# Softmax finished in its selection's step, and filling matmuls, in a fused attention, MLP and expert kernel

## The reference, cut to what matters

```python
def _attn_ref(q, k, v):                        # batch 4, 8 heads, 576 rows, head 64
    scores = scale * np.matmul(q, k.transpose(0, 1, 3, 2))
    kth = np.partition(scores, -32, axis=-1)[..., -32:-31]
    scores = np.where(scores >= kth, scores, -1000000000.0)
    attn = np.exp(scores - np.max(scores, axis=-1, keepdims=True))
    attn = attn / (np.sum(attn, axis=-1, keepdims=True) + 1e-09)
    return np.matmul(attn, v)

def _moe_ref(x, w_in, w_out):                  # 2304 tokens, 512 -> 2048 -> 512
    h = x @ w_in
    return (np.maximum(h, 0.0) + np.log1p(np.exp(-np.abs(h)))) @ w_out

def _moe2_ref(x, w_gate, w1, w2):              # best of 8 experts for each token, 512 -> 1024 -> 512
    ...
    ye = np.maximum(xe @ w1[e], 0.0) @ w2[e]
    out[mask] = gate_w[mask, None] * ye
```

## Time and profile before

| | |
|---|---|
| median of 3 runs | 1057.04 us (1056.1 to 1057.84) |
| the profiled execution | 1057.04 us |
| its span | 1054.8 us |
| mean granted clock of TensorE | 0.983 |
| busy: TensorE, VectorE, ScalarE, GpSimd | 992.9, 817.3, 727.6, 711.9 us |
| HBM | 123 GB/s over the span |

### The profile page before, as it was taken

How to read it: one execution, slowest core, us unless ns; L and a number is a source line. 1 busy time by engine, 2 the same in 40 slices (tenths; PEclk the granted TensorE clock), 3 DMA queues, 4 the chain that set the end, 5 groups by cost and what they waited for, 6 DMA issues and landing times.

```text
span 1054.8 us, 21596 instructions
## 1 busy us (share of the span) xinstructions
PE 992.9 (94%) x6878; PEld 806.3 (76%) x6879; DVE 817.3 (77%) x1744; ACT 727.6 (69%) x1390; POOL 711.9 (67%) x831
## 2 busy tenths in 40 slices
PE   5565899999999999999999999999999999999996
PEld 2343687788788788788788888887887788888875
DVE  7999999999999999999999999994345622222261
ACT  3888898988998998998888999998554111111140
POOL 2688898889899899899888899899351311111101
PEclk9996899999999999999999999999999999999999
DMA  9723253343344343324434333333481421111100
GB/s 311 257 91 127 112 171 121 128 143 121 114 153 165 114 157 121 124 98 144 169 119 155 117 120 102 121 121 121 156 331 54 165 96 52 40 40 40 40 20 20
DMA packets 43391, 130.99 MB, mean 124 GB/s; under 512 B 4320, under 2 KB 18656, under 8 KB 33056
## 3 DMA queue, kind: packets, MB, share of 16 engines
q1 hardware_dynamic: 40256, 120.09, 32.5%
q0 software_dynamic: 3040, 9.70, 2.7%
HBM read 111.95 MB, written 18.09 MB: 123 GB/s over the span
## 4 chain that ended last, share of the span: by engine, by line
PE 80%; DVE 8%; POOL 4%; ACT 3%; issue 3%; DMA 1%; SPq 1%; ACTq 0%; DVEq 0%; POOLq 0%
PE psum L614 8%; PE psum L575 7%; PE psum L644 7%; PE psum L737 6%; PE psum L739 6%; PE psum L738 6%; PE psum L646 6%; PE psum L645 6%; PE psum L663 6%; PE psum L665 6%; PE psum L664 6%; PE psum L589 5%; DVE top L1158 3%; DVE work L1164 3%; PE psum L769 2%
## 5 line engine op out<-in xcount | busy, mean ns | idle before, releaser
L1158 DVE MAX8 top<-work 128x8 f32<-128x576 f32 x432 | 305.4, 752 | 0.0
L1164 DVE MATCH_REPLACE8 work<-top,work 128x576 f32<-128x576 f32 x288 | 212.6, 749 | 0.0
L644 PE MATMUL psum<-x_parts,wi_hi 128*128 128x256 f32 x576 | 171.1, 297 | 0.0
L645 PE MATMUL psum<-x_parts,wi_hi 128*128 128x256 f32 x576 | 162.9, 283 | 0.0
L646 PE MATMUL psum<-x_parts,wi_lo 128*128 128x256 f32 x576 | 162.7, 283 | 0.0
L614 PE MATMUL psum<-prT,vtok 128*64 128x128 f32 (+3 forms) x1600 | 117.1, 287 | 15.2 <-ACT prT L918 15.2
L614 PEld LDWEIGHTS psum<-prT,vtok 128*64 128x64 f32 (+1 forms) x1600 | 85.5, 144 | 54.2 <-issue 41.2
L575 PE MATMUL psum<-kT,qT 64*128 64x512 f32 (+3 forms) x640 | 113.0, 480 | 11.5 <-DMA qT<-in_q 4.4
L1638 POOL DMA_INDIRECT out<-ys,dst_now x19 | 19.2, 1012 | 152.6 <-DVE ys L1360 150.7
L663 PE MATMUL psum<-wo_ring,h_hi 128*128 x288 | 119.1, 414 | 1.0 <-POOL h_lo L1547 0.9
L1541 POOL TENSOR_TENSOR hs<-hs,ab 128x512 f32<-128x512 f32 x72 | 93.7, 1301 | 32.7 <-ACT ab L941 32.5
(11 more groups left out here) (215 smaller groups left out, 2353.1 us busy)
## 6 DMA issues: line engine op xcount, KB each, us to landing
wo_ring<-wo_parts SPq DMA_DIRECT2D x72, 1024.0 KB, 4.8
wo_parts<-wo_ring SPq DMA_DIRECT2D x8, 1024.0 KB, 3.8
kT<-in_k SPq DMA_DIRECT2D x16, 288.0 KB, 3.4
qT<-in_q SPq DMA_DIRECT2D x16, 288.0 KB, 3.9
vtok<-in_v SPq DMA_DIRECT2D x16, 256.0 KB, 2.9
wo_raw<-in_moe_w_out SPq DMA_DIRECT2D x1, 4096.0 KB, 14.1
wi_raw<-in_moe_w_in SPq DMA_DIRECT2D x4, 1024.0 KB, 14.4
x_rows<-x2tok SPq DMA_DIRECT2D x16, 256.0 KB, 2.4
```

What stands on the lines that cost most here:

```text
L644: nc.tensor.matmul(ps[:, part, :], wi_hi[:, u, kk, f], hi, start=first, stop=False)
L645: nc.tensor.matmul(ps[:, part, :], wi_hi[:, u, kk, f], lo, start=False, stop=False)
L1158: nc.vector.max(top[:, at, 8 * r:8 * r + 8], sc_of(n)[:, t, :] if r == 0 else work[:, t, :]).then_inc(topk_step, 1)
L1164: nc.vector.match_replace(work[:, t, :], top[:, at, 8 * r - 8:8 * r], sc_of(n)[:, t, :] if r == 1 else work[:, t, :], TAKEN).then_inc(topk ...
```

## The change

- The steps before the MLP (`i < MLP_AT`): ScalarE does `probs_out(i - 2)` first, then the cut-offs, `split_wo`, the exponentials of `i - 1`, `x_out(i - 2)`, `scores_out`, and in the same step `normalise(i - 1)`, then `split_wi`. TensorE turns block `i - 2` at once, multiplies it by V, and takes the scores last.
- From step 10: scores are two blocks ahead, since step 9 has none. ScalarE does the exponentials of block `i - 2` at the start of step `i`, with `x_out(i - 3)` between the two tiles, ahead of `scores_out` and `h_high`.
- GpSimd: `biases(i - 1)` comes to the start of its own step, `softplus(i)`, `x_split_up(i - 2)`, `denominators(i - 1)` and `h_low(i)` follow the masks.
- The row's reciprocal is no longer made by VectorE, but by GpSimd, as `den` to the power of -1, behind `den`. VectorE has the selection alone.
- Block 8 is cut by ScalarE in both tiles (`FREE` is 9 in place of 8).
- `w_out` is loaded by two DMAs in place of one, and `split_wo` waits for its half.
- TensorE: in steps 5 to 9, four products of the identity by itself behind the transposes, and in 5 to 8 fourteen behind the scores. Nobody reads them.

```diff
-        def scores_at(i):
-            return i + 1 if i <= 0 else i + AHEAD
+        def scores_at(i):
+            return i + 1 if i <= 0 else i + 3 if i < MLP_AT - 1 else i + 2 if i >= MLP_AT else BLOCKS
+
+        def scores_made(i):
+            return min(i + 4, MLP_AT + 2) if i < MLP_AT else min(i + 3, BLOCKS)
...
+            def fill(i, many):
+                if MLP_AT - 5 <= i < MLP_AT:
+                    for _ in range(many):
+                        nc.tensor.matmul(psum[:, 7, 0:P], ident[:], ident[:], start=True, stop=True)
...
+                if i < MLP_AT:
+                    if late:
+                        turn_probs(i - 2, scores_made(i - 1))
+                        fill(i, 4)
+                        times_v(i - 2)
+                    if is_block(n):
+                        scores(n, max(i - 1, 0))
+                        fill(i, 14)
...
+                behind = late and i > MLP_AT
+                if behind:
+                    exponentials(i - 2, 0)
+                if is_block(i - 3) and i > MLP_AT:
+                    x_out(i - 3)
+                if behind:
+                    exponentials(i - 2, 1)
+                if is_block(scores_at(i)):
+                    scores_out(scores_at(i))
                 if up_at(i - 1):
                     h_high(*up_at(i - 1))
...
             def denominators(n):
                 pool.wait_ge(exp_ready, 2 * n + 2)
                 if n >= 2:
-                    pool.wait_ge(rden_ready, n - 1)
+                    pool.wait_ge(pr_ready, 2 * n - 2)
                 nc.gpsimd.tensor_tensor(den[:, n % 2, :], eps[:, n % 2, :, 0], eps[:, n % 2, :, 1],
                                         ALU.add).then_inc(den_step, 1)
+                pool.wait_ge(den_step, n + 1)
+                nc.gpsimd.tensor_tensor(rden[:, n % 2, :], den[:, n % 2, :], inverse[:], ALU.pow
+                                        ).then_inc(rden_ready, 1)
```

More of the change, by code:

```diff
@@ L455, in _ @@
                 load_v(0, p)
-            sp.dma_start(wo_raw[:], w_out.rearrange("(k p) n -> p k n", p=P)).then_inc(wo_loaded, 16)
+            for half in range(2):
+                at = slice(half * KF // 2, (half + 1) * KF // 2)
+                sp.dma_start(wo_raw[:, at, :], w_out.rearrange("(k p) n -> p k n", p=P)[:, at, :]
+                             ).then_inc(wo_loaded[half], 16)
             for kk in range(KD):
@@ L578, in scores, with turn_probs @@
                 mm.then_inc(scores_ready, 1)
-            def turn_probs(n):
+            def turn_probs(n, made):
                 if n:
@@ L583, in turn_probs @@
                     pe.wait_ge(x_copied, n)
-                pe.wait_ge(scores_copied, 2 * min(scores_at(n + 2) + 1, BLOCKS))
+                pe.wait_ge(scores_copied, 2 * made)
                 for t in range(2):
@@ L1040, in _ @@
                     if late:
[L1041 to L1044, removed]
+                        probs_out(i - 2)
                     if now:
@@ L1052, in _ @@
                         exponentials(i - 1, 0)
+                    if late and i == MLP_AT - 1:
+                        x_out(i - 2)
+                    if now:
                         exponentials(i - 1, 1)
-                    if late:
-                        probs_out(i - 2)
-                    if wi_unit(i) is not None:
-                        split_wi(wi_unit(i))
+                    if late and i < MLP_AT - 1:
+                        x_out(i - 2)
+                    if is_block(scores_at(i)):
+                        scores_out(scores_at(i))
                     if i == 0:
@@ L1060, in _ @@
                         scores_out(scores_at(i) + 2)
-                    continue
+                    if now:
+                        normalise(i - 1, 0)
+                        normalise(i - 1, 1)
+                    if wi_unit(i) is not None:
+                        split_wi(wi_unit(i))
+                    continue
+                behind = late and i > MLP_AT
[5 more added lines that the diff above has]
+                    exponentials(i - 2, 1)
+                if is_block(scores_at(i)):
+                    scores_out(scores_at(i))
                 if up_at(i - 1):
                     h_high(*up_at(i - 1))
-                if is_block(i - 3):
-                    x_out(i - 3)
-                if now:
-                    for t in cuts(i - 1):
-                        cut_off(i - 1, t)
-                if is_block(scores_at(i)):
-                    scores_out(scores_at(i))
-                if late:
+                if behind:
                     normalise(i - 2, 0)
@@ L1077, in _ @@
                     probs_out(i - 2)
+                if now:
+                    for t in cuts(i - 1):
+                        cut_off(i - 1, t)
                 if i in TURNS:
```

86 lines of the change are left out of this document (40 added, 46 removed).

## The result

The changed kernel takes 1084.8 us (median of 4 runs, 1084.75 to 1085.34), the kernel before on the same chip 1056.89 us. The ratio is 1.0265, 95% interval 1.0247 to 1.0283: **slower by 28 us**. The forecast was 1062.6 with a range of 1052 to 1076. The sign was right, the size was not, and the range does not hold the time.

What follows compares the result with a forecast made beforehand. The prediction took TensorE's own work to bound the middle, with GpSimd nearest behind. Entry -3.2, middle +5.1 and last steps +3.7 gave +5.6 us on 1057.04, so 1062.6 us, with a range of 1052 to 1076.

Steps and rivals of the forecast that it cites:

- The power's price: GpSimd's new power on 128x2 elements, without a row: taken as 0.36 us, between bounds of 0.193 and 0.46.
- Rival C: The power is dear: from 0.5 us GpSimd is slower than TensorE's mean; 1071 at 0.6, 1083 at 0.8; chance 0.13.
- GpSimd's round: GpSimd's work per step without waits: grows from 9.45 by 0.41 to 9.86 us, 9.69 and 9.96 at the bounds.
- The entry: Steps before and at the MLP's start: step 13 starts at 135.3, 3.2 us earlier (4.7 and 2.3 at the bounds).
- Up to normalise(7): First stretch of the entry: from split_wi(0) at 38.72, normalise(2) at 47.3 and normalise(7) at 98.0, against 98.91 before.
- The ring's sum: Steps 1 to 9, waits joining ScalarE and GpSimd: 9.57 us plus the power, 9.93 us a round.
- Steps 11 and 12: End of the entry: step 11 at 113.4, power of block 10 at 129.4, transposes wait 2.6 us, step 13 at 135.3.
- the wait at 38.72: Entry: split_wi(0) waits for its weights until 38.72, covering the wait that loading w_out in halves removes.
- The middle: TensorE's steps in the MLP loop: h_low starts at 2.95 at best, the power must end by 3.45; 5.1 us later.
- The margin and the boundary steps: Middle: margin 0.5 us, short steps use 0.41 each; 1.05 us at four group boundaries, 0.3 at three, 5.1 later.
- The last steps: Steps 70 to 73: 38.5 us for 36.03; with one more block of scores behind step 13, 3.7 us later.
- Rival A: The margins hold: no waits at group boundaries, entry gives 4.7 to 5.8, last steps take 1.2 to 2.0; 1052.5 to 1054.5; chance 0.25.

Runs made afterwards that it cites:

- e_dve: The changed kernel with the reciprocal back on VectorE in place of GpSimd's power, order otherwise kept; 1072.7 us, ratio 1.0154 to the kernel before.
- e_old_pow: The kernel before, in its own order, with GpSimd's power behind den replacing VectorE's reciprocals from block 9; 1066.7 us, ratio 1.0096.
- e_ln: The changed kernel with the reciprocal made by ScalarE as exp(-ln(den)) ahead of normalise; 1087.6 us, ratio 1.0294 to the kernel before.
- the best kernels: e_best, e_best_fill, and the latter with VectorE's reciprocal of block n - 2 ahead of block n's first maxima; 1053.8, 1054.1 and 1053.3 us.
- the exchange: ScalarE makes h_high ahead of scores_out from step 10; alone on the changed kernel, power included, 1070.4 us, ratio 1.0134 to the kernel before.
- e_best: The changed kernel with h_high ahead of scores_out and the reciprocals on VectorE, placed early in its selection; 1053.8 us, ratio 0.9976 to before.
- e_best_fill: e_best with filling products in step 10 too, ten ahead of the wait for x and four ahead of the products with V; 1054.1 us.

## Why the prediction was wrong, step by step

**The power's price: wrong, and its bound too.** 0.36 was taken, 0.46 was the upper bound; it is 0.721. The bound came from "the nearest dearer one", a subtraction of 64 times as many elements. A subtraction's time bounds no power's. The forecast weighed the small reciprocal on VectorE, 0.165 us; the power is 4.4 times that. The Trainium skill (GPSIMD Engine Reference, Performance versus the Vector engine) puts GpSimd's elementwise work at about half of VectorE's speed; an estimate by it was 0.33 us. The trace agrees with it in neither: the sum is 0.195 us on GpSimd and 0.144 as VectorE's TENSOR_REDUCE in the first blocks of the kernel before, 1.35 times, and the power 4.4 times the reciprocal. Rival C had half of the mechanism: "from a power of 0.5 us GpSimd is slower than TensorE's mean everywhere". The case was named with its time (1071 at 0.6, 1083 at 0.8) and a chance of 0.13, far too low for an operation without a row; the range ended at 1076, inside it. That 1084.8 lies next to its 1083 is luck. By its own working a power of 0.721 puts step 13 at 138.5 and 61 rounds of 10.22 behind it, which gives 1077 (and at 0.6 some 1069, not 1071); the ring and the later entry, which it has not, make up the rest.

**GpSimd's round: right in its form, a little high.** The forecast's 9.45 + 0.05 + power gives 10.22 at 0.721; measured 10.05 to 10.07.

**The entry: forecast 3.2 earlier, measured 4.9 later.** Three stretches were each too short in it, 8.1 us together.
- *Up to normalise(7)*, 101.28 for 98.0. The ring's sum was right in form: 9.93 - 0.36 + 0.72 = 10.29, measured 10.26 in steps 7 to 9. Six powers at 0.36 more are 2.2 of the 3.3 us. The rest lies ahead of normalise(2), which starts at 48.66 for 47.3: `split_wi(0)` is 0.24 us later, and the forecast's chain goes straight on to `probs_out(1)`, but this waits 0.73 us for transposes at the low clock's pace (1.94 us for eight, 1.23 later).
- *From there to step 11*, 17.7 us for 15.4. The forecast has no low clock in step 10. There are no filling products in it, TensorE waits, the granted clock falls to 0.50, and the products with V take 2.60 us for 1.46. That is 1.1 of the 2.3 us, and the power of block 8 is 0.36; the rest was not followed up.
- *Steps 11 and 12*, 24.4 us for 21.9. Scores at the low clock (granted 0.50 from 119 to 122 us, 2.40 us for 1.30) come late, `scores_out` behind them, `h_high` behind that, and GpSimd's `h_low` waits 1.74 us at 123.26. The power of block 10 comes at 135.01, forecast 129.4.

```profile
116.45 2.60 PE L624 MATMUL psum<-prT,vtok 128*64 128x128 f32 x20 [1.21 <-ACT prT L944]
```

```profile
123.26 1.30 POOL L1568 TENSOR_TENSOR h_lo<-hs,h_hi 128x512 fp32r<-128x512 f32 x1 [1.74 <-ACT h_hi L975]
```

The halves of `w_out`, which in the forecast the wait at 38.72 "covers", are worth 3.5 us at step 13. Without them `split_wi(0)` of the changed kernel starts at 43.66, not at the forecast's 38.72.

**The middle: a ring was missing.** The forecast said `h_low` "starts at 2.95 at best", from the scores, their copy and `h_high`. It took for granted that ScalarE reaches `scores_out` as soon as TensorE has the scores. But the diff puts `exponentials(i - 2, 1)` ahead of it, which waits for the second mask in GpSimd's list; in e_dve `h_low` starts 3.58 us into the step (342.07, the step from 338.49). The forecast's own sentence, that the moved calls "alter what waits for what", was the right question and was not worked through on ScalarE. The ring costs 10.3 us by itself (e_dve), the power 10.8 by itself (e_old_pow), and both 24.8, so 3.7 come only of the two together.

**The margin and the boundary steps: right kind, wrong number.** Short steps and group boundaries were to be late by 1.05 us a group, 5.1 in all. Step 26 takes 10.57 for 10.05 (forecast 10.84), the step behind it 10.76 for 9.94, and the groups between steps 18 and 66 lose 2.4 to 3.3 each. The margin itself, the latest start of `normalise` that TensorE does not notice, was read rightly, as e_ln shows.

**The last steps: right in form.** Four steps take 41.0 us for 36.03; forecast 38.5. Four rounds of GpSimd at the measured 10.05 are 40.2.

**Rival A** (the margins hold) is what the best kernels do: 134.5 to 134.9 at step 13, 739 at step 74, and 1053.3 to 1053.8 us, inside the 1052.5 to 1054.5 that it was given. It needed a reciprocal that costs GpSimd nothing, and the exchange. Its terms are off both ways: in e_best the entry gives 3.6 us (forecast 4.7 to 5.8) and the last four steps take 36.1 for 36.0 (forecast 1.2 to 2.0 more).

The gap between the forecast and the profiled execution, 22.7 us, is thus: entry 8.1, middle and last steps 16.0, less 1.4 behind step 74.

## What to carry to other kernels

When a list of calls is reordered, write down for each engine what now stands ahead of a call that others wait for, and follow it back until it closes: a ring of 9.8 us in a step of 9.45 costs time although every engine has idle time. Two calls exchanged gave back 14 us here, and a cheap operation in place of the power no more than 20 up to step 74. There can be more than one ring, and the same work costs more in the one that has no room: 0.49 us on ScalarE, off the first ring, cost more than 0.72 on GpSimd. And an operation without a row in the trace has no upper bound in the rows of other operations; run it once before a plan rests on it.

## What the hardware showed unexpectedly

- GpSimd's two-input instruction on 128x2 takes 0.195 us as sum or as product, and 0.721 us as power. At the same shape the operation makes a factor of 3.7.
- ScalarE's logarithm and exponential of 128x2 take 0.22 and 0.20 us: together less than the power, but they stood between the scores and the transposes, where TensorE had no time left.
- Products of the identity that nobody reads kept TensorE at its high clock and took 3.39 us for fourteen, in pauses that were there anyway (the forecast had 2 us for them at the high clock). In step 10 they kept it too (e_best_fill), and gained nothing, since another engine set the end.
